# Group sums over two token tiles at a time, and a store chunk's rows dealt to two DMA engines instead of three

## The reference

```
kv = k^T v                      per batch (8) and head (8), 64 x 64, over 576 positions
o  = q kv;  x = o / sqrt(mean(o*o) + 1e-6) * g_norm        -> x: 4608 tokens x 512
logits = x phi                  4608 x 32 (8 experts x 4 slots)
d = exp(logits - max over tokens); d /= sum over tokens + 1e-9
slot_input = d^T x              32 x 512, a sum over all 4608 tokens
slot_out[e] = relu(slot_input[e] w1[e]) w2[e]              8 experts, 512 -> 1024 -> 512
c = softmax over the 32 slots of logits;  out = c slot_out -> 4608 x 512
```

## Time and profile before

| | us |
|---|---|
| median of 3 runs | 173.69 |
| the three runs | 173.69, 172.13, 173.83 |
| the profiled execution | 172.27 |
| its span, first to last instruction | 170.92 |

### The profile page before, as it was taken

The page is one execution under the profiler, slowest core; times in us unless marked ns, Lnnn a source line. Parts: engine busy times, 40 slices in busy tenths (PEclk is TensorE's granted clock), DMA queues, the critical chain, the costliest instruction groups (busy, mean ns, idle before and its releaser), DMA issues.

```text
span 170.9 us, 4509 instructions
## 1 busy us (share of the span) xinstructions
PE 148.6 (87%) x1971; PEld 108.2 (63%) x1971; DVE 85.9 (50%) x184; ACT 88.9 (52%) x230; POOL 59.5 (35%) x72
## 2 busy tenths in 40 slices
PE   7988897989999899999899998999999889989200
PEld 3467766979788888898797785355566443555000
DVE  1122166283677265762936798724897037118300
ACT  3027576786975887768749864203214046217300
POOL 6000708548357755467482679400000004000000
PEclk9999999999999999999999999999999999999955
DMA  5999999999999999999999999999999999999995
GB/s 188 420 425 432 437 416 433 482 415 481 414 427 412 457 427 428 414 397 460 426 429 418 437 428 414 443 420 422 429 426 437 466 399 426 405 427 424 437 443 253
DMA packets 4302, 71.67 MB, mean 419 GB/s; under 512 B 726, under 2 KB 726, under 8 KB 858
## 3 DMA queue, kind: packets, MB, share of 16 engines
q1 hardware_dynamic: 3994, 71.18, 97.6%
q0 software_dynamic: 288, 0.20, 0.4%
HBM read 61.94 MB, written 9.44 MB: 418 GB/s over the span
## 4 chain that ended last, share of the span: by engine, by line
PE 48%; DMA 24%; ACT 12%; DVE 7%; SPq 2%; issue 1%
PE psum L214 48%; DMA arena<-in_kv_dram 13%; DMA arena<-in_w_dram 10%; ACT bd L214 3%; ACT sq L214 3%; ACT xall L214 2%; SPq L214 2%; DVE arena L214 1%; DVE logits L214 1%; ACT arena L214 1%; DVE ms L214 1%; ACT part L214 1%; ACT d L214 1%; DVE part L214 1%; ACT r L214 1%
## 5 line engine op out<-in xcount | busy, mean ns | idle before, releaser
L214 PE MATMUL psum<-bd,arena 128*128 128x192 f32 (+1 forms) x320 | 56.1, 335 | 1.9 <-ACT bd L214 1.5
L214 PEld LDWEIGHTS psum<-bd,arena 128*128 128x128 f32 (+1 forms) x320 | 45.4, 179 | 7.1 <-ACT bd L214 2.8
L214 DVE TENSOR_REDUCE ms<-sq 128x16 f32<-128x1024 f32 (+1 forms) x19 | 22.1, 1162 | 32.7 <-ACT sq L214 32.4
L214 POOL TENSOR_TENSOR part<-part,r 128x512 f32<-128x512 f32 x17 | 17.8, 1048 | 49.8 <-DVE r L214 49.8
L214 POOL TENSOR_TENSOR xall<-xall,r 128x512 f32<-128x512 f32 x34 | 34.7, 1042 | 0.0
L214 ACT ACTIVATE sq<-psum 128x512 f32<-128x512 f32 x36 | 21.5, 598 | 12.5 <-PE psum L214 12.3
L214 PE MATMUL psum<-arena 128*64 128x64 f32 (+1 forms) x640 | 21.7, 226 | 2.6 <-DMA arena<-in_kv_dram 2.1
L214 PEld LDWEIGHTS psum<-arena 128*64 128x64 f32 (+1 forms) x640 | 19.0, 137 | 7.2 <-DMA arena<-in_kv_dram 3.6
L214 ACT COPY xall<-psum 128x512 f32<-128x512 f32 x34 | 20.7, 608 | 0.0
L214 ACT COPY part<-psum 128x256 f32<-128x256 f32 (+1 forms) x38 | 13.7, 359 | 11.8 <-DVE part L214 10.7
L214 DVE TENSOR_REDUCE logits<-part 128x64 f32<-128x512 f32 (+1 forms) x18 | 17.8, 990 | 0.0
(11 more groups left out here) (76 smaller groups left out, 125.4 us busy)
## 6 DMA issues: line engine op xcount, KB each, us to landing
arena<-in_w_dram SPq DMA_DIRECT2D x4, 4096.0 KB, 23.8
arena<-in_w_dram SPq DMA_DIRECT2D x4, 2048.0 KB, 20.7
arena<-in_t_dram SPq DMA_DIRECT2D x1, 6912.0 KB, 35.9
arena<-in_w_dram SPq DMA_DIRECT2D x2, 3072.0 KB, 22.6
arena<-in_kv_dram SPq DMA_DIRECT2D x2, 2304.0 KB, 23.4
arena<-in_kv_dram SPq DMA_DIRECT2D x1, 4608.0 KB, 42.6
arena<-in_kv_dram SPq DMA_DIRECT2D x1, 3584.0 KB, 32.2
arena<-in_kv_dram SPq DMA_DIRECT2D x3, 1152.0 KB, 13.2
```

Of the source, the lines that this page charges most:

```text
L214: inst = getattr(engine, method)(*args, **kwargs)
```

## The change

- `group_sum` takes two tiles of a group at once. For tile i + a (a is 0 or 1) and j of 0 and 1, one product takes blocks j and j + 2 of the tile together, 258 moving columns, and goes to rows 64a + 32j of a PSUM tile of 128 x 258. There are 4 products for two tiles, where there were 8. `acc` has 258 columns.
- The two tiles' halves of `acc` (rows 0 to 63 and 64 to 127) are added when it is transposed: `psT` is made by two products with `fold` (two identities of 64, one above the other) and a third of one column that gives the sum of d. `rs` is read from `psT`.
- `fold` is made at the start, one more reduction on VectorE and one more copy on GpSimd; `sel` is made from its own first block. `eps`, `run_max` and `rs` become columns of one small tile.
- The outermost dimension of the 24 rows' piece is 2 instead of 3, and the second `step_over` is 6 instead of 5. In the author's words: the second chunk's 24 rows over GpSimd's queue on engines 7 and 8, twelve each, none on 9.

```diff
-    ("gpsimd", 1, 4, 24, 3, 1, 1, 2), ("gpsimd", 97, 4, 8, 2, 1, 1, 2),
+    ("gpsimd", 1, 4, 24, 2, 1, 1, 2), ("gpsimd", 97, 4, 8, 2, 1, 1, 2),
-STEPS = (7, 5)
+STEPS = (7, 6)
...
+    fold = const.tile([P, 2, 64], F32, name="fold")
+    nc.vector.tensor_reduce(out=fold[:, 0], in_=ident.rearrange("p (g n) -> p n g", g=2), axis=AX.X, op=ALU.add)
     sel = const.tile([P, 4, NS], F32, name="sel")
-    nc.gpsimd.tensor_copy(out=sel, in_=sel32.unsqueeze(1).to_broadcast([P, 4, NS]))
+    nc.vector.tensor_reduce(out=sel[:, 0], in_=ident.rearrange("p (g n) -> p n g", g=4), axis=AX.X, op=ALU.add)
+    nc.gpsimd.tensor_copy(out=sel[:, 1:], in_=sel[:, :1].to_broadcast([P, 3, NS]))
...
+    nc.gpsimd.tensor_copy(out=fold[:, 1], in_=fold[:, 0])
...
-    acc = const.tile([P, 129], F32, name="acc")
+    acc = const.tile([P, 258], F32, name="acc")
...
         if i == 0:
-            sums[G] = ps.tile([P, 129], F32, tag="s", name=f"pS{G}")
+            sums[G] = ps.tile([P, 258], F32, tag="s", name=f"pS{G}")
         pS = sums[G]
-        x = xts[(g0[G] + i) % NX]
-        for j in range(4):
-            nc.tensor.matmul(
-                pS[32 * j : 32 * j + 32], lhsT=ds[G][:, i], rhs=x[:, j], start=i == 0, stop=i == GROUPS[G] - 1
-            )
-        if i == GROUPS[G] - 1:
+        for a in range(2):
+            x = xts[(g0[G] + i + a) % NX]
+            for j in range(2):
+                at = 64 * a + 32 * j
+                nc.tensor.matmul(
+                    pS[at : at + 32].rearrange("p (j n) -> p j n", n=129),
+                    lhsT=ds[G][:, i + a],
+                    rhs=x[:, j::2],
+                    start=i == 0,
+                    stop=i == GROUPS[G] - 2,
+                )
+        if i == GROUPS[G] - 2:
...
-            todo_sums += [(sums_at[T], i) for i in range(GROUPS[sums_at[T]])]
-        for _ in range(min(2, len(todo_sums))):
+            todo_sums += [(sums_at[T], i) for i in range(0, GROUPS[sums_at[T]], 2)]
+        if todo_sums:
             group_sum(*todo_sums.pop(0))
...
-    psT = ps.tile([P, P], F32, tag="m", name="psT")
-    nc.tensor.transpose(psT, acc[:, :128], ident)
+    psT = ps.tile([P, P + 1], F32, tag="m", name="psT")
+    for j in range(2):
+        nc.tensor.matmul(
+            psT[:, 64 * j : 64 * j + 64], lhsT=acc[:, 129 * j : 129 * j + 128], rhs=fold[:, 0], start=True, stop=True
+        )
+    nc.tensor.matmul(
+        psT[:, 128:129], lhsT=fold.rearrange("p a n -> p (a n)"), rhs=acc[:, 128:129], start=True, stop=True
+    )
...
-    nc.vector.tensor_scalar_add(rs, acc[:, 128:129], EPS_SUM)
+    nc.vector.tensor_scalar_add(rs, psT[:, 128:129], EPS_SUM)
```

More of the change, by code:

```diff
@@ L368, in soft_moe_linear_attention @@
     stepped = const.tile([P, 16], F32, name="stepped")
-    eps = const.tile([P, 1], F32, name="eps")
+    small = const.tile([P, 4], F32, name="small")
+    eps = small[:, :1]
     nc.gpsimd.memset(eps, EPS_RMS)
-    sel32 = const.tile([P, NS], F32, name="sel32")
-    nc.vector.tensor_reduce(out=sel32, in_=ident.rearrange("p (g n) -> p n g", g=4), axis=AX.X, op=ALU.add)
+    fold = const.tile([P, 2, 64], F32, name="fold")
+    nc.vector.tensor_reduce(out=fold[:, 0], in_=ident.rearrange("p (g n) -> p n g", g=2), axis=AX.X, op=ALU.add)
     sel = const.tile([P, 4, NS], F32, name="sel")
-    nc.gpsimd.tensor_copy(out=sel, in_=sel32.unsqueeze(1).to_broadcast([P, 4, NS]))
+    nc.vector.tensor_reduce(out=sel[:, 0], in_=ident.rearrange("p (g n) -> p n g", g=4), axis=AX.X, op=ALU.add)
+    nc.gpsimd.tensor_copy(out=sel[:, 1:], in_=sel[:, :1].to_broadcast([P, 3, NS]))
     gphi = const.tile([P, 2, 2, 2, NS], F32, name="gphi")
@@ L390, in pos @@
         return T + T // GROUPS[0] + 1
-    run_max = [const.tile([P, 1], F32, name=f"rmax{i}") for i in range(2)]
-    acc = const.tile([P, 129], F32, name="acc")
+    run_max = [small[:, 1 + i : 2 + i] for i in range(2)]
+    acc = const.tile([P, 258], F32, name="acc")
     def pool(**tags):
@@ L767, in soft_moe_linear_attention @@
     group_exp(G - 1)
-    todo_sums += [(G - 1, i) for i in range(GROUPS[G - 1])]
+    todo_sums += [(G - 1, i) for i in range(0, GROUPS[G - 1], 2)]
     mean_square(s - 1)
@@ L795, in soft_moe_linear_attention @@
     fill(LATE_FILL[2], home=tail_ps[:, 1], cols=512)
-    for i in range(GROUPS[G]):
+    for i in range(0, GROUPS[G], 2):
         group_sum(G, i)
@@ L802, in soft_moe_linear_attention @@
     nc.gpsimd.memset(sTe, 0.0)
-    psT = ps.tile([P, P], F32, tag="m", name="psT")
-    nc.tensor.transpose(psT, acc[:, :128], ident)
+    psT = ps.tile([P, P + 1], F32, tag="m", name="psT")
[6 more added lines that the diff above has]
+    )
     fill(LATE_FILL[4], home=tail_ps[:, 1], cols=512)
-    mine = psT.rearrange("p (j e k) -> p e j k", j=4, k=SPE)
+    mine = psT[:, :P].rearrange("p (j e k) -> p e j k", j=4, k=SPE)
     last = NE - 1
@@ L817, in soft_moe_linear_attention @@
     )
-    rs = const.tile([P, 1], F32, name="rs")
-    nc.vector.tensor_scalar_add(rs, acc[:, 128:129], EPS_SUM)
+    rs = small[:, 3:4]
+    nc.vector.tensor_scalar_add(rs, psT[:, 128:129], EPS_SUM)
     nc.vector.reciprocal(rs, rs)
```

## The result

| | before | after |
|---|---|---|
| median, us | 173.61 | 172.04 |
| runs, us | 172.13 to 174.11 (8 runs) | 171.97 to 172.38 (8 runs) |
| profiled execution, us | 172.27 | 171.97 |
| its span, us | 170.92 | 170.60 |

The ratio of the times is 0.9916, with an interval of 0.9896 to 0.9936: faster by 0.8%. The forecast was 172.0. Of before's eight runs one lies at 172.13 and seven at 173.5 or more; the eight of after lie within 0.41 us. So the median fell by 1.57 us, while the lowest runs of the two kernels differ by 0.16 and the two profiled executions, both near the lowest, by 0.30. Two gains have to be explained: the small one in every execution, and 1.3 us that most executions of before lose and none of after does.

What follows compares the result with a forecast made beforehand. The kernel was taken as a queue of bytes for 16 DMA engines, ended by whichever finishes last; 172.27 - 0.25 (rows), all else zero, gave 172.0 us, also taken as median, eight in ten from 171.5 to 173.8.

Steps and rivals of the forecast that it cites:

- the case that was held likeliest: End of the last store: the last engine is relieved, median near 172.0 us (171.5 to 172.4); chance 0.47.
- The rows of chunk 1: End of the DMA queue: eight rows less on engine 9, four more on 7 and 8; -0.25 us, from +0.94 to -0.4.
- The choice between the bounds: Last store: engine 9 taken to end alone (0.25 us earlier), rather than 7 or 8 (0.94 us later).
- R1: End of the last store: engine 7 or 8 ends last, 173.2 us against the profiled time, 174.6 against the median; chance 0.12.
- From there to the median: Step from the profiled execution to the runs' median: 172.0 us taken as likeliest, though the spread may stay.
- The candidate: Cause of the runs' spread: one more instruction-code packet on the engine that ends alone, 0.91 us.
- Case B: Median: same gain of 0.25 us, but runs go on spreading, median between 172.0 and 173.5 us; chance 0.33.
- Instruction code: TensorE's code on the DMA queue: one packet fewer, 0 to -0.91 us on the last engine, taken as 0.
- Group sums on TensorE: Six tiles' products: 9.2 us if columns set the pace, 4.6 if instructions do; worth nothing, hidden by the DMA queue.
- Folding and transposing: VectorE's `acc` fold +0.13 us a group, transpose +0.7 us; tail about 0.8 us later, hidden by 9.8 us of queue.
- Start: Kernel's start: extra reduction (0.37 us) and copy hidden behind the first load's wait; zero, +0.4 us without that cover.

Runs made afterwards that it cites:

- the profiled high run: The kernel before, unchanged, run and profiled once more: 173.61 us median of 12 runs, ratio 1.0015; the profiled execution took 174.05 us.
- the sums alone: After with the old deal of the 24 rows (eight each on engines 7, 8 and 9), keeping the new group sums: 173.5 us, ratio 1.0008.
- the kernel with 8: After with 7 more idle fill products ahead of the first expert, which starts 1.2 us later: 173.02 us, ratio 0.9956.
- 17: After with 16 more idle fill products ahead of the first expert, which starts 3.1 us later: 173.45 us, ratio 1.0006.

## Why the prediction was right

The forecast median, 172.0, came out (172.04), and by the case that was held likeliest. Step by step:

- **The rows of chunk 1: right.** The term was -0.25 us for an execution like the profiled one; the two profiled executions differ by 0.30, their spans by 0.32, which is the size of the gap that the last packets showed. The choice between the bounds was right too: engine 9 is the one that ended alone (the rows on 8 and 9: 174.35), and 7 and 8 have room for twelve rows. R1 is refuted by the change itself and by the 0.2 to 0.4 us that both still have to spare. The rule that speaks for R1 (the Trainium skill, "DMA: Bandwidth & Descriptors", section "Latency and other measured facts": engines 7 and 15 usually slower) is not borne out here, 172.55 with sixteen rows on 7 against 172.73 on 8. The Trainium skill's rule on the turn in which a GpSimd transfer takes its engines (same page, "Why a DMA increments its semaphore by 16 and not by 1") agrees as far as times can tell: one step of the cursor brought rows back to the late engine, 174.35 for 172.04.
- **From there to the median: right in kind, too small in size, and in part luck.** The candidate was one more packet of code on the engine that ends alone, at 0.91 us. It is that: the late engine of the profiled high run carries two packets of code, the place of that engine comes up twice in the four high executions profiled with a full queue and once in the low one, and without its rows the high runs are gone at 14 or 15 packets. But 0.91 could not carry the 1.35 us between the runs. The packet costs its engine 0.94 itself and 0.5 more on the data packet behind it. Against this stand 1.88 us of rows taken off the engine. It ended 0.25 behind the next one, so by these figures it now ends 1.6 us ahead of it with one packet, and 0.2 ahead with two: last in neither. The prediction had no row for what sets the levels and priced the packet by half a microsecond too little; that eight rows outweigh it even so is luck. Case B, a gain with the runs still spreading, is refuted by 171.97 to 172.38.
- **Instruction code: right.** 14 packets for 15, and worth nothing: the sums alone have 14 and take 173.5. By the turn of eight it only makes the low runs likelier, two in eight for one in eight; 9 of 36 and 16 of 116 were.
- **Group sums on TensorE: right, at the upper bound.** Columns set the pace; six tiles take 1.52 us for 1.53, and all of them 10.8 us as before.
- **Folding and transposing: right in size, wrong in their cover.** Forecast were +0.13 a group and 0.8 us at the tail, measured 0.14 and 0.76. The cover was named as 9.8 us of queued transfers, with stores bound by weights for 17.72 us behind it. Both were misread. The piece of 17.72 us in the chain is the duration of a transfer, and TensorE waited for it 0.7 us; the queue held 6.5 us; and a delay of the tail goes on to the stores, where some 1.7 us are covered. What hid the 0.76 us was the 0.7 us of waiting, which it replaced, so that the stores moved by 0.09. With some two and a half times the delay (the kernel with 8) the median is 1.0 us higher, though not four of its twelve runs, and with five times (17) 1.4 us: there the argument would have failed.
- **Start: right**, as far as the total tells; nothing of it shows in the span.

## What to carry to other kernels

When a kernel is one full queue of bytes, the engine that ends last is the whole case: read the last store's packets in short windows, and count everything that the late engine carries, packets of instruction code included. If runs of one kernel fall on two levels, profile one of each; the difference may be one packet on one engine, and the cure is to leave that engine a packet's worth less. A DMA piece in the chain of waits is a transfer's duration; how long an engine waited for it stands in the waits, and only that much, with the slack of the last stores, covers a delay.

## What was not expected of the hardware

- A packet of TensorE's instruction code (16 KB) costs the DMA engine that carries it about 1.4 us, 0.94 for itself and 0.5 on the next data packet, and eight engines take these packets in turns that start elsewhere from one execution to the next: 1.35 us between the runs of one kernel. The Trainium skill, "Runtime: NRT & Kernel Launch", section "Instruction fetch mechanics", has such blocks of 256 instructions fetched as the program runs, at a cost mostly hidden; the counts agree (15, 14 and 8 packets with 3942, 3664 and 2064 products and loads), the hidden cost does not where the DMA engine that carries one is the last to end. The turn of eight is read from the packets' lengths and from packets followed back, eight apart on one engine; no view names a packet's engine.
- Products with 32 weight columns cost the same with 258 moving columns at once as with twice 129: 1.52 and 1.53 us for six tiles. Fewer weight loads, 3.2 for 7.0 us, gained nothing.
- With a delay of 1.2 us ahead of the experts the clock fell to 1.2 GHz some 30 us later, in the execution profiled, and cost 1.3 us there; after, without the delay, kept 2.4 GHz in that stretch. That the delay brought it about is not shown.
